# Attention followed by a top-1 expert layer: the experts' weights asked for by ScalarE instead of SyncE

## The reference

```
out_up    = repeat(softmax attention over means of 4 rows, 4)
out_local = softmax attention in a band |i - j| < 4
x         = (out_up + out_local) as rows of 512      # 4 x 576 = 2304 tokens
logits    = x @ w_gate ; local = sigmoid(x @ w_local)
e[s]      = argmax(logits[s]) if s == 0 or local[s] < 0.5 else e[s-1]
out[s]    = softmax(logits[s])[e] * (relu(x[s] @ w1[e]) @ w2[e])
```

## Time and profile before

| | |
|---|---|
| three runs | 456.43 us median (455.15 to 458.4) |
| the profiled execution | 456.83 us |
| its span, first to last instruction | 455.1 us |
| PE busy | 422.9 us |
| DVE busy | 307.9 us |
| ACT busy | 226.9 us |
| DMA | 93.76 MB, mean 206 GB/s |
| mean granted clock of PE | 0.972 of full speed |

### The profile page before, as it was taken

How to read it: one execution, slowest core, us unless ns; L and a number is a source line. 1 busy time by engine, 2 the same in 40 slices (tenths; PEclk the granted TensorE clock), 3 DMA queues, 4 the chain that set the end, 5 groups by cost and what they waited for, 6 DMA issues and landing times.

```text
span 455.1 us, 13398 instructions
## 1 busy us (share of the span) xinstructions
PE 422.9 (93%) x3901; PEld 337.8 (74%) x3908; DVE 307.9 (68%) x506; ACT 226.9 (50%) x397; POOL 309.4 (68%) x324
## 2 busy tenths in 40 slices
PE   7999999999999557999999999999999989799993
PEld 3888888888778334778888888888877868588872
DVE  5678788887766786875863964783495776738440
ACT  3777778777766203262634545353454637334210
POOL 7878787777989704787876775787387577674411
PEclk9999999999999858999999999999999999899997
DMA  7979999998625568358779677969869697584430
GB/s 168 200 166 195 202 190 196 183 199 176 206 60 142 140 170 328 108 157 245 260 245 325 216 229 235 320 187 304 275 183 347 236 295 263 171 295 137 152 103 33
DMA packets 105738, 93.76 MB, mean 206 GB/s; under 512 B 49431, under 2 KB 84247, under 8 KB 105689
## 3 DMA queue, kind: packets, MB, share of 16 engines
q1 hardware_dynamic: 99960, 81.91, 65.3%
q0 software_dynamic: 5728, 11.30, 8.1%
HBM read 71.66 MB, written 22.82 MB: 208 GB/s over the span
## 4 chain that ended last, share of the span: by engine, by line
PE 75%; DVE 7%; DMA 7%; issue 4%; SPq 3%; POOL 2%; ACT 1%; DVEq 0%; POOLq 0%; ACTq 0%
PE psum L1630 43%; PE psum L1360 5%; DMA h_rows<-tile_bufs 5%; PE psum L1433 4%; PE psum L1448 3%; PE psum L1396 3%; PE psum L1462 2%; PE psum L1370 2%; PE psum L1526 2%; PE psum L1419 2%; POOL tile_bufs L726 2%; PE psum L1409 2%; PE psum L1537 2%; PE psum L1342 2%; SPq L504 1%
## 5 line engine op out<-in xcount | busy, mean ns | idle before, releaser
L726 POOL DMA_INDIRECT tile_bufs<-x_rows,from_part x96 | 122.7, 1278 | 60.3 <-DVE x_raw L1237 32.0
L1630 PE MATMUL psum<-w_ring,h_t 128*128 x552 | 134.1, 399 | 5.5 <-DVE w_ring L1223 4.8
L1630 PE MATMUL psum<-w_ring,xg_t 128*128 x552 | 131.2, 393 | 0.5 <-issue 0.3
L1630 PEld LDWEIGHTS psum<-w_ring,h_t 128*128 128x128 f32 x552 | 104.6, 190 | 31.9 <-issue 6.9
L1630 PEld LDWEIGHTS psum<-w_ring,xg_t 128*128 128x128 f32 x552 | 103.5, 188 | 24.8 <-issue 1.5
L1223 DVE TENSOR_TENSOR w_ring<-w_ring (+1 forms) x28 | 63.6, 2292 | 27.5 <-ACT w_ring L892 20.0
L892 ACT CAST w_ring<-w_ring (+1 forms) x28 | 52.0, 1906 | 49.3 <-DMA w_ring<-moe_w 47.8
L1249 DVE STREAM_TRANSPOSE h_raw<-h_part 128x512 f32<-128x512 f32 x46 | 30.0, 689 | 40.1 <-DMA h_part<-h_rows 40.1
L929 ACT CAST h_t<-h_raw 128x512 fp32r<-128x512 f32 x46 | 27.1, 622 | 55.7 <-DVE h_raw L1249 55.6
L921 ACT ACTIVATE tile_bufs<-psum 128x512 f32<-128x512 f32 x46 | 24.9, 593 | 51.4 <-PE psum L1630 48.2
L732 POOL DMA_INDIRECT out<-tile_bufs,to_row x23 | 29.2, 1270 | 24.5 <-DVE tile_bufs L1264 19.0
(11 more groups left out here) (187 smaller groups left out, 608.3 us busy)
## 6 DMA issues: line engine op xcount, KB each, us to landing
w_ring<-moe_w SPq DMA_DIRECT2D x28, 1024.0 KB, 8.8
h_rows<-tile_bufs SPq DMA_DIRECT2D x46, 256.0 KB, 2.7
h_part<-h_rows SPq DMA_DIRECT2D x92, 128.0 KB
early<-q SPq DMA_DIRECT2D x32, 144.0 KB, 3.9
early<-k SPq DMA_DIRECT2D x32, 144.0 KB, 4.0
early<-v SPq DMA_DIRECT2D x16, 288.0 KB
x_rows<-early SPq DMA_DIRECT2D x48, 96.0 KB, 2.5
early<-v SPq DMA_DIRECT2D x32, 120.0 KB
```

Source lines behind the costliest of these rows:

```text
L726: pool.indirect_dma_start(xg[:, t % 2, s * 128:(s + 1) * 128], None, x_parts[:, :], bass.IndirectOffsetOnAxis(from_part[:, t, s:s + 1], 0) ...
L1630: ins = mm(bank[b][:, :], rows, w_ring[:, bass.ds(at + (off + c * width + n * 512), 512)], start=(c == 0 and k == 0), stop=(c == chunks - ...
```

## The change

ACT, not SP, issues the loads of the experts' weights. After the change SP issues only the stores and reads of h in the stage of the products. ACT issues both pieces of w1 right after relu(t) and both pieces of w2 at the end of its tile, after a wait for S(t-2) when there is something to load. The loads of expert 1 come from ACT, at the place in its stream where it used to wait for their landing. DVE forms both remainders of w2 at the end of tile t, and nothing is left for tile t+1. In the routing, slots are kept as whole numbers and rounded to a multiple of 128 by adding 1.5 * 2^30, so that `row_iota` needs no subtraction; the table is written by POOL after the remainders of expert 0, and DVE waits for it (`s_rows`) ahead of L1181.

```
-        WHOLE = 1.5 * 2.0 ** 23
+        WHOLE = 1.5 * 2.0 ** 23 * SLOTS
...
+        s_rows = sem("s_rows")
...
         @block.sync
-            def load_w1(e, at, piece, par): ...
-            def load_w2(e, at, piece, par): ...
...
-            for b in range(NB):
-                sp.wait_ge(s_xrow[b], 16 * NS)
-            sp.wait_ge(s_xt, LGROUPS * KD)
-            for i in range(PIECES):
-                load_w1(1, PLACE, i, 0)
-            for i in range(PIECES):
-                load_w2(1, PLACE, i, 0)
...
             h_store(0, 0)
             h_back(0, 0)
+            h_store(1, 1)
+            token_weights()
+            h_back(1, 1)
+            for t in range(2, SURE):
+                h_store(t, t % 2)
+                h_back(t, t % 2)
             sp.wait_ge(s_tabs, 2)
-            e, at = next_of(1)
-            load_next(load_w1, s_w1_in, 1, e, at, 0, PIECES)
-            tile(1, 1, w2=False)
-            for t in range(2, SURE):
-                tile(t, t % 2)
...
                 with sp.If(used > t):
-                    tile(t, t % 2, w1=(t < MT - 1))
+                    h_store(t, t % 2)
+                    h_back(t, t % 2)
...
         @block.gpsimd
-                step(nc.gpsimd.iota(tile_iota[:], [[1, MT], [0, TILES]], base=0, channel_multiplier=0,
+                step(nc.gpsimd.iota(tile_iota[:], [[SLOTS, MT], [0, TILES]], base=0, channel_multiplier=0,
                                     allow_small_or_imprecise_dtypes=True))
-                step(nc.gpsimd.iota(row_iota[:], [[1, SLOTS], [0, TILES]], base=0, channel_multiplier=0,
-                                    allow_small_or_imprecise_dtypes=True))
-                step(nc.gpsimd.tensor_scalar(row_iota[:], row_iota[:], -(SLOTS - 1) / 2, None, ALU.add))
...
             constants()
             for i in range(2, FPIECES):
                 first_lo(i)
+            nc.gpsimd.iota(row_iota[:], [[1, SLOTS], [0, TILES]], base=0, channel_multiplier=0,
+                           allow_small_or_imprecise_dtypes=True).then_inc(s_rows, 1)
...
         @block.scalar
+            def load_w1(e, at, piece, par):      # as SP's was, with act.dma_start
+            def load_w2(e, at, piece, par):
...
+            def load_next(t, load, s_in, par, s_free=None, free=None):
+                e = act.value_load(tab_next[0:1, one(t)], min_val=0, max_val=E - 1)
+                with act.If(e != 0):
+                    if s_free is not None:
+                        wait(act, s_free, free)
+                    at = act.value_load(tab_next_w[0:1, one(t)], min_val=0, max_val=PLACE)
+                    for place in (0, PLACE):
+                        with act.If(at == place):
+                            for i in range(PIECES):
+                                load(e, place, i, par)
+                with act.If(e == 0):
+                    act.sem_inc(s_in[par], 16 * PIECES)
...
+            for b in range(NB):
+                act.wait_ge(s_xrow[b], 16 * NS)
+            act.wait_ge(s_xt, LGROUPS * KD)
+            for i in range(PIECES):
+                load_w1(1, PLACE, i, 0)
+            for i in range(PIECES):
+                load_w2(1, PLACE, i, 0)
             split_hi(s_w1_in[0], s_w1_hi, 1, PLACE, W1C)
...
             act.wait_ge(s_tabs, 2)
+            load_next(1, load_w1, s_w1_in, 1)
             relu(1, 1)
+            load_next(2, load_w1, s_w1_in, 0)
             h_hi(0, 0)
...
                 relu(t, par)
+                if w:
+                    load_next(t + 1, load_w1, s_w1_in, 1 - par)
                 h_hi(t - 1, 1 - par)
                 if x:
                     x_hi(t + 2, par)
                 if w:
                     split_next_hi(t, half + 1, s_w1_in[par], s_w1_hi, 0, W1C)
                 split_next_hi(t - 2, half, s_w2_in[par], s_w2_hi, W1C, W2C)
+                load_next(t - 1, load_w2, s_w2_in, 1 - par, s_y, t - 1)
...
         @block.vector
-            step(V.scalar_tensor_tensor(slot[:], slot[:], -(SLOTS + 1) / 2, slot_base[:], ALU.add, ALU.add))
-            step(V.tensor_scalar(slot_big[:], slot[:], 1.0 / SLOTS, WHOLE, ALU.mult, ALU.add))
+            step(V.scalar_tensor_tensor(slot[:], slot[:], -1.0, slot_base[:], ALU.add, ALU.add))
+            step(V.tensor_scalar(slot_big[:], slot[:], -(SLOTS - 1) / 2, WHOLE, ALU.add, ALU.add))
             step(V.tensor_scalar(slot_tile[:], slot_big[:], -WHOLE, None, ALU.add))
-            step(V.scalar_tensor_tensor(slot_row[:], slot_tile[:], -float(SLOTS), slot[:], ALU.mult, ALU.add))
+            step(V.tensor_tensor(slot_row[:], slot[:], slot_tile[:], ALU.subtract))
...
+            dve.wait_ge(s_rows, 1)
             for n in range(0, TILES, HOT):
...
-                if late:
-                    split_next_lo(t - 3, s_w2_hi, s_w2, W1C, W2C, 1, PIECES)
                 y_scale(t - 2, par, half)
                 if w:
                     split_next_lo(t, s_w1_hi, s_w1, 0, W1C)
-                split_next_lo(t - 2, s_w2_hi, s_w2, W1C, W2C, 0, 1)
+                split_next_lo(t - 2, s_w2_hi, s_w2, W1C, W2C)
```

More of the change, by code:

```diff
@@ L505, in h_back, with token_weights @@
                                  h_rows[par].rearrange("(s i) (a n) -> a i s n", s=QUADS, a=QUADS)[a]).then_inc(s_hp, 16)
[L507 to L529, removed]
+            def token_weights():
+                sp.wait_ge(s_weight_t, 1)
+                for s in range(2):
+                    sp.dma_start(w_rows.rearrange("(n s p) o -> s n (p o)", s=2, p=QS)[s],
+                                 weight_t[:, 64 * s:64 * s + QS]).then_inc(s_wrow, 16)
             h_store(0, 0)
             h_back(0, 0)
-            sp.wait_ge(s_tabs, 2)
-            e, at = next_of(1)
-            load_next(load_w1, s_w1_in, 1, e, at, 0, PIECES)
-            tile(1, 1, w2=False)
-            for t in range(2, SURE):
-                tile(t, t % 2)
+            h_store(1, 1)
[4 more added lines that the diff above has]
+                h_back(t, t % 2)
+            sp.wait_ge(s_tabs, 2)
             used = sp.value_load(tab_end[0:1, E - 1:E], min_val=1, max_val=MT)
@@ L777, in _ @@
         def _(act):
+            w1v = w1.rearrange("e (c p) f -> e p c f", p=128)
+            w2v = w2.rearrange("e (c p) d -> e p c d", p=128)
+            def load_w1(e, at, piece, par):
+                n = KD // PIECES
+                act.dma_start(w_ring[:, at + WCOLS + piece * n * F:at + WCOLS + (piece + 1) * n * F].bitcast(F32).rearrange(
+                                 "p (c f) -> p c f", c=n),
+                             w1v[one(e), :, piece * n:(piece + 1) * n, :].rearrange("o p c f -> p (o c) f")
+                             ).then_inc(s_w1_in[par], 16)
+            def load_w2(e, at, piece, par):
+                n = KF // PIECES
+                act.dma_start(w_ring[:, at + WCOLS + W1C + piece * n * D:at + WCOLS + W1C + (piece + 1) * n * D].bitcast(F32).rearrange(
+                                 "p (c d) -> p c d", c=n),
+                             w2v[one(e), :, piece * n:(piece + 1) * n, :].rearrange("o p c d -> p (o c) d")
+                             ).then_inc(s_w2_in[par], 16)
             def tr_out(g, u, par):
@@ L1224, in split_lo, with split_next_lo @@
                                             ALU.subtract).then_inc(s_lo, 1)
-            def split_next_lo(t, s_hi, s_lo, at, cols, first=0, end=PIECES):
+            def split_next_lo(t, s_hi, s_lo, at, cols):
                 e = dve.value_load(tab_next[0:1, one(t)], min_val=0, max_val=E - 1)
@@ L1230, in split_next_lo @@
                     split_lo(s_hi, s_lo, e,
-                             dve.value_load(tab_next_w[0:1, one(t)], min_val=0, max_val=PLACE) + at, cols, first, end)
+                             dve.value_load(tab_next_w[0:1, one(t)], min_val=0, max_val=PLACE) + at, cols)
             def x_tr(t, par, came):
@@ L1265, in y_scale, with tile @@
                                         ALU.mult).then_inc(s_y_out, 1)
-            def tile(t, par, half, x=True, w=True, late=True):
+            def tile(t, par, half, x=True, w=True):
                 h_tr(t - 1)
@@ L1314, in _ @@
             split_lo(s_w2_hi, s_w2, 1, PLACE + W1C, W2C)
-            tile(2, 0, 0, late=False)
-            tile(3, 1, 0, late=False)
+            tile(2, 0, 0)
+            tile(3, 1, 0)
             with dve.Fori(2, SURE // 2) as m:
```

17 lines of the change are left out of this document (2 added, 15 removed).

## The result

The changed kernel takes 466.51 us (median of 4 runs, 464.1 to 467.79) against 457.26 us (4 runs, 455.15 to 458.4) of the kernel before beside it: ratio 1.0164, 95% interval 1.0113 to 1.0216. It is **slower** where I forecast faster, by between 1.1 and 2.2 per cent, and lies 12.0 us above the top of the range. The profiled executions took 467.79 and 456.83 us, 10.96 apart.

A forecast was written before the change was run, and what follows sets the result against it. PE was taken to set the pace, with time to regain only where it stalls: 6.88 us in the products plus 1.39 in the routing, 8.27 off 456.83, gives 448.56, median 448.2; range 446.3 to 454.5.

The forecast's parts named there:

- The place of the gain: Products' stage, F(17) to F(20): PE's waits for `w_ring` at S(15) and S(17) vanish, gaining 6.88 us with the clock.
- Weights from ACT: Tight stretch of the products: ACT issues loads sooner than SP; expert 6's w2 lands near 379 instead of 382.37.
- What waits behind ACT. Cost: nothing: ACT's queue: a load's 2.6 us delays relu and h_hi at no cost, unless ACT is already about 5 us late.
- Issue time of expert 6's w2: ACT's queue in the products: w2 of expert 6 issued at about 365.5, 3.5 us before the old 369.07.
- One pass: DVE forms both w2 remainders ahead of h_tr; this or sooner issue alone removes most of the wait; together 6.88 us.
- My lower bound: If w2's landing did not move, S(17) still waits 1.4 us and the products save 3.6 us.
- The table: Routing: L1119 on DVE takes 0.36 instead of 1.75 us, and S(0) begins sooner by a gain of 1.39 us.
- my lower bound of 0.65: Routing: if the first gather lands no sooner, at least the 0.65 us PE waited at S(0) for h is gained.
- B: Half the gain: h and weights share DMA engines, landing times stay; 451.4 us, or 452.2 without routing's gain; chance 0.18 with E.
- E: ACT's loads might enter the same queue as SP's stores; same time as B; chance 0.18 together with B.
- D: Issuing blocks ACT until an earlier load lands, 14 us lost over experts 5 to 7: 462 us; chance 0.09 with other slower ways.
- C: A wait of ACT's takes the place in tiles 15 to 17, h_hi(17) late: 453.5 us at best, up to 456; chance 0.13.

The follow-up runs named there:

- after_third: The changed kernel unaltered, run once more in another group: 478.1 us against 476.47 of the kernel before, ratio 1.002.
- only_act: The kernel before with the weight loads issued by ACT and nothing else changed: 481.28 us against 476.09, ratio 1.012.
- sp_loads_3: Third run of the changed kernel with weight loads back in SP's queue in the old order: 472.54 us, ratio 1.0005 to the kernel before.
- before_again: The kernel before, unaltered, run again for a trace in the slower conditions: ratio 1.0036.
- small_act: The changed kernel with loads of experts 2 to 7 cut to an eighth of the columns: 451.28 us against 458.51 of the kernel before, ratio 0.9852.
- act_behind_h: The changed kernel with ACT's load of the next w1 moved behind h_hi and x_hi: 467.83 us against 458.51 of the kernel before, ratio 1.0218.
- after_again: The changed kernel unaltered, run again for a second trace: 464.33 us against 458.51 of the kernel before, ratio 1.0125.
- sp_loads: The changed kernel with weight loads back in SP's queue in the old order, run three times: ratios 0.9929, 0.9954 and 1.0005 to the kernel before.
- sp_act_order: The changed kernel with loads back on SP, both w1 pieces ahead of h's reads: 474.68 us, ratio 0.9939 to the kernel before; rerun 470.91, 0.9946.

## Why the prediction was wrong

**The place of the gain.** It was read rightly: the waits of S(15) and S(17) for `w_ring` went, and the quiet stretch before 339 us hardly changed.

**The step that failed** is in "Weights from ACT" and in "What waits behind ACT. Cost: nothing". I took the slow store of 12.46 us to be cured by taking the weights out of its queue, and kept the speed of all else. In place of this the store's leg of tiles 14 and 16, short before, grew (5.23 to 6.96, 3.70 to 7.44 us) and the reading leg grew most (6.95 to 12.10, 7.11 to 10.54). I had written "as long as ACT isn't already about 5 us late": relu(16) was 10.1 us behind the end of F(16), for 3.3 us before (350.93 + 5.76 against 359.99 of the earlier trace rows). The 2.6 us that I gave a load on ACT, covered by F(t+1), were 3.98 for expert 6's w2, and relu(17) was 4.8 us behind F(17), 2.1 of them after the store of h(16) had landed. I looked at the one store that was slow and not at those that were quick because the order had put them ahead of the weights. The Trainium skill ("DMA: Bandwidth & Descriptors", Queues, rings and completion order) says that each DMA engine takes turns between its queues, a packet at a time; under that rule a second queue gives weights a turn beside every transfer of h. The trace agrees as far as it goes, by the two legs of tile 14; no run here shows the turns themselves.

**Issue time of expert 6's w2.** Forecast 365.5, 3.5 us sooner than before. It was 378.72, since ACT, which now issues it, had been held by h. The loads were to come sooner by leaving SP, and came later because ACT waits in the loop of h.

**One pass.** No harm and no gain by itself (0.9997 twice), where I said each move alone would take most of the wait away. With the loads on ACT it does help: 2.2 us of waits for `w_ring` in `after_third`, 9.9 in `only_act`. My lower bound held S(17) to 1.4 us; in `sp_loads_3` it still waits 2.40, and 1.90 in `before_again`.

**The table.** The contention was read rightly: 1.75 us became 0.36. It is not the edit alone that does this. DVE in `before_again`, with the old table, in a late head:

```profile
157.56 0.36 DVE L1119 TENSOR_TENSOR e_buf<-logits,lmax 112x192 f32<-112x192 f32 x1
```

POOL's last remainder ended at 156.44 there, ahead of the subtraction, which is short. What failed is the path from there to S(0): `small_act` and `act_behind_h` have S(0) at 199.76 and 199.70 against 200.03, 0.3 us sooner, and `after_again` at 200.79; not 1.39, and under my lower bound of 0.65. In `small_act` the gather left 1.15 us sooner (174.67 against 175.82), but PE had its rows at 181.12 against 181.01. In all twenty traces these rows reach PE 13.9 to 14.6 us after the first of expert 1's loads (166.71 before), while the gather itself leaves 7.3 to 9.1 us after it. So the rows seem to come when those 4 MB are through, however early the gather leaves; no run here changes these loads alone to show it. The wait at 128 us is there in `before_again` too (1.53 us), with S(0) at 201.99 beside the changed kernel's 201.89, so the late head of the profiled execution is no part of the change.

**The rivals.** B's premise, that landing times stay as they were, was too kind: they did not for h. E is false, by q10. D's price was near (462), but its mechanism is false: an issue on ACT took 0.40 us. C was closest: a wait of ACT's did take the place. I let it do no more than eat the gain; it came in other tiles, was larger than the waits removed, and fed on itself over two tiles. A loop that grows had no case among mine, and so no place in the range.

**What stays open.** Whether the second queue, the moments at which the weights now leave, or ACT's own time for them does the harm: no run has the one without the others, as SP in one queue cannot ask for w1 at ACT's moment without standing ahead of the store. Also why the changed kernel lost 1.2 to 1.6% in two groups of runs and 0.2% in a third. No version tried is surely faster than the kernel before: `sp_loads` was clear of it once in three times, and `sp_act_order` came to 0.994 and 0.995.

## What to carry to other kernels

Before bulk loads get a queue of their own, list the small transfers in the loop that feeds the busy engine, and beside each write which load stands ahead of it now and which will run beside it then: an order in one queue can be what keeps them quick. Do not judge by the one slow transfer alone. And be wary of letting an engine issue bulk loads which itself waits in that loop: here its lateness reached the loads, the roundings and the next round at once, though no run shows what this alone costs.

## What the runs showed of the hardware

- Two hardware queues were served together: with 2 MB of w1 and 2 MB of w2 in the one, the store and read-back of 0.5 MB of h's rows in the other took 19.1 us, against 9.3 with an eighth of the weights (tile 14).
- The same kernel took 457 and 476 us in different groups of runs; in the slower ones PE waited in 10 to 22 places for "issue" (9.1 us in 13 places in `before_again`; in the products of the profile before, one such wait of 0.27 us).
- The first gather on GpSimd took 5.1 us to land where it left 9.1 us behind the first of expert 1's 4 MB of loads (before), and 6.3 us where it left 7.4 to 7.8 us behind it (`act_behind_h`, `after_again`, `small_act` and the changed kernel).
- A subtraction on DVE of two operands of 112x192 in SBUF took 1.75 us where GpSimd was writing remainders, 0.36 us where it was through, with the old table too (`before_again`).
- An ACT issue of a 1 MB load took 0.40 us in the median, between 330 and 410 us 0.42 at most, with 2 to 4 MB under way.
